# Copies of the first two attention states on ACT instead of DVE, and the four chunk scans of the late stabiliser at other unit ends

## What is computed

```python
for t in range(S):
    m_new = np.maximum(f_gate[:, :, t] + m, i_gate[:, :, t])
    f_stab, i_stab = np.exp(f_gate[:, :, t] + m - m_new), np.exp(i_gate[:, :, t] - m_new)
    C = f_stab * C + i_stab * outer(v_t, k_t);  n = f_stab * n + i_stab * k_t
    y[:, :, t] = o * (C q_t) / np.maximum(abs(n . q_t), 1.0)
x  = (silu(xn @ w_gate) * (xn @ w_val)) @ w_out        # xn: RMS-normalised y, d_ff = 1536
out = (sigmoid(x @ w_gate2) * (x @ w_val2)) @ w_out2
```

## Time and profile before

| | us |
|---|---|
| median of three runs | 469.57 |
| the profiled execution | 469.45 |
| its span | 467.7 |
| PE busy | 458.5 |
| DVE busy | 226.1 |
| ACT busy | 184.6 |
| POOL busy | 26.8 |

### The profile page before, as it was taken

How to read it: one execution, slowest core, us unless ns; L and a number is a source line. 1 busy time by engine, 2 the same in 40 slices (tenths; PEclk the granted TensorE clock), 3 DMA queues, 4 the chain that set the end, 5 groups by cost and what they waited for, 6 DMA issues and landing times.

```text
span 467.7 us, 7890 instructions
## 1 busy us (share of the span) xinstructions
PE 458.5 (98%) x3067; PEld 378.0 (81%) x3067; DVE 226.1 (48%) x451; ACT 184.6 (39%) x379; POOL 26.8 (6%) x59
## 2 busy tenths in 40 slices
PE   8899999999999999999999999999999999999997
PEld 4588898888888887888888888888888888888885
DVE  5898658876666553645555452222322222322222
ACT  6755546553542342354444552222322222322222
POOL 4411111111010000000000000000000000000000
PEclk9999999999999999999999999999999999999999
DMA  7565026620210300002222200000000000100001
GB/s 217 186 193 145 22 96 204 178 86 15 72 36 24 125 2 0 2 1 95 95 97 95 83 0 0 2 0 1 32 24 1 0 1 0 57 1 0 1 0 57
DMA packets 15837, 26.30 MB, mean 56 GB/s; under 512 B 2264, under 2 KB 10808, under 8 KB 15800
## 3 DMA queue, kind: packets, MB, share of 16 engines
q1 hardware_dynamic: 15576, 25.68, 17.7%
q10 hardware_dynamic: 224, 0.12, 0.1%
HBM read 23.55 MB, written 1.97 MB: 55 GB/s over the span
## 4 chain that ended last, share of the span: by engine, by line
PE 90%; DVE 4%; issue 3%; ACT 1%; POOL 1%; DMA 1%; DVEq 0%; POOLq 0%; ACTq 0%
PE bank L1373 53%; PE bank L1435 7%; PE bank L1437 7%; PE bank L1436 7%; PE bank L1443 3%; PE bank L1444 3%; PE pair L1313 2%; PE pair L1290 2%; PE bank L1380 1%; PE pair L1327 1%; PE pair L1279 1%; PE bank L1345 1%; PE bank L1360 1%; DMA fi_row<-fi_first 1%; DVE x_lo L1027 0%
## 5 line engine op out<-in xcount | busy, mean ns | idle before, releaser
L1373 PE MATMUL bank<-x_hi,gv_split 128*128 128x512 f32 (+1 forms) x780 | 236.6, 374 | 1.4 <-DVE hid L1052 0.8
L1373 PEld LDWEIGHTS bank<-x_hi,gv_split 128*128 128x128 f32 x780 | 143.1, 188 | 28.2 <-issue 2.4
L1373 PE MATMUL bank<-x_lo,gv_split 128*128 128x512 f32 (+1 forms) x436 | 161.4, 373 | 0.0
L1065 DVE TENSOR_TENSOR hid<-hid,bank 128x512 f32<-128x512 f32 x48 | 33.0, 687 | 132.4 <-PE bank L1373 132.4
L625 ACT ACTIVATE hid_hi<-hid 128x512 fp32r<-128x512 f32 (+1 forms) x78 | 46.6, 598 | 123.0 <-DVE hid L1065 90.6
L1373 PEld LDWEIGHTS bank<-x_lo,gv_split 128*128 128x128 f32 x436 | 82.0, 188 | 14.1
L618 ACT ACTIVATE hid<-bank 128x512 f32<-128x512 f32 (+1 forms) x78 | 43.9, 562 | 119.1 <-PE bank L1373 88.7
L1072 DVE TENSOR_TENSOR hid_lo<-hid,hid_hi 128x512 fp32r<-128x512 f32 (+1 forms) x78 | 51.1, 655 | 42.1 <-ACT hid_hi L625 42.1
L1435 PE MATMUL bank<-hid_hi,wo_split 128*128 128x512 f32 (+1 forms) x154 | 59.7, 388 | 0.0
L1437 PE MATMUL bank<-hid_hi,wo_split 128*128 128x512 f32 (+1 forms) x154 | 57.5, 374 | 0.0
L1436 PE MATMUL bank<-hid_lo,wo_split 128*128 128x512 f32 (+1 forms) x154 | 57.5, 373 | 0.0
(11 more groups left out here) (165 smaller groups left out, 358.0 us busy)
## 6 DMA issues: line engine op xcount, KB each, us to landing
gv_raw<-wgv SPq DMA_DIRECT2D x24, 384.0 KB, 3.1
qk_tile<-qk SPq DMA_DIRECT2D x24, 160.0 KB
wo_raw<-wo SPq DMA_DIRECT2D x24, 160.0 KB, 3.2
v_sb<-v SPq DMA_DIRECT2D x12, 168.0 KB, 4.6
gate<-og SPq DMA_DIRECT2D x12, 160.0 KB, 3.5
k_sb<-k SPq DMA_DIRECT2D x10, 160.0 KB, 4.7
outT<-y_out SPq DMA_DIRECT2D x6, 256.0 KB, 2.0
rhs<-log_split SPq DMA_DIRECT2D x16, 4.0 KB
```

The costliest lines, as they stand in the source:

```text
L1065: ins = nc.vector.tensor_tensor(h, h, v_ps[:, 0:size], ALU.mult)
L1373: mm = pe.matmul(ps[:, 0:size], lhs, rhs, start=(i == 0), stop=whole and i == len(passes) - 1)
```

## The change

DVE no longer copies states 0 and 1; ACT does it with an activation of kind Copy. `first_state(0)` stands in unit 0 behind round_hidden(0) and before round_wo(1); `first_state(1)` stands in unit 1 behind activate(1) and before gate_tanh(2). The scans of chunks 2, 3, 4, 5 stand at the ends of units 1, 1, 3, 3 instead of 0, 0, 1, 3. All that stands ahead of unit 0 is the same.

```diff
-SCAN_AT = (0, 0, 1, 3)
+SCAN_AT = (1, 1, 3, 3)
...
+            def first_state(t):
+
+                act.wait_ge(st_done, t + 1)
+                nc.scalar.activation(state[t][:], st_ps[:, 0:HG * DV].rearrange("p (h d) -> p h d", h=HG),
+                                     ACT.Copy).then_inc(state_done, 1)
...
                 activate(u)
+                if u == 1:
+                    first_state(1)
...
                     round_hidden(u)
+                if u == 0:
+                    first_state(0)
...
                 sums = st_ps[:, 0:HG * DV].rearrange("p (h d) -> p h d", h=HG)
-                if t < B:
-                    nc.vector.tensor_copy(state[t][:], sums).then_inc(state_done, 1)
-                else:
-                    dve.wait_ge(decayed, t - B + 1)
-                    dve.wait_ge(att_out, 2 * t + 2)
-                    nc.vector.tensor_tensor(state[t % B][:], sums, faded[:], ALU.add).then_inc(state_done, 1)
+                dve.wait_ge(decayed, t - B + 1)
+                dve.wait_ge(att_out, 2 * t + 2)
+                nc.vector.tensor_tensor(state[t % B][:], sums, faded[:], ALU.add).then_inc(state_done, 1)
...
-                if u == 1:
-                    update_state(1)
...
-                if u == 0:
-                    update_state(0)
```

## The result

The changed kernel takes 468.85 us in the median (468.73 to 469.08), the kernel before 469.52 in the runs made beside it; the ratio is 0.9984, 95% interval 0.9978 to 0.9990. That is 0.67 us less. The forecast was 0.5 us less (469.1 us; 0.25 to 0.7 won). The interval leaves out 1, so the changed kernel is the faster one, but by about 0.15% only, less than the 0.2% that the prediction held to be tellable. The profiled span went from 467.7 to 467.0 us.

The account below looks back on a forecast made before the run. DVE sets the pace from 26 to 48 us, then PE alone. Unit 6 starts at 51.22 instead of 51.80, 0.58 us won; less 0.1 for collisions, 0.5: 469.57 - 0.5 = 469.07, written 469.1 us, range 468.4 to 469.8.

Parts of the forecast that it names:

- The frame: Start of unit 6 on PE: how much earlier it comes is the change's worth; everything behind it moves along.
- Part 1: Copies leave DVE: 0.2 us won at state 0, about 0.06 at state 1; PE 0.88 earlier, called the larger gain.
- Part 2: Copies on ACT: 0.35 us each, bounds 0.2 and 0.4, both covered by ACT's waiting and so costing nothing.
- Part 3: Two first scans leave unit 0, a 0.90 us step on DVE: combine(2) at about 30.75, 0.95 us earlier.
- Part 4: Ends of units 1 and 3, one scan more each: 0.50 us hidden in unit 1's following hole, 0.50 given back in unit 3.
- Part 5: Unit 6 on PE: the later of PE's arrival, 51.15, and the x_hi path, 51.22, counts; gain 0.58 us.
- What can eat some of it: POOL's unit 1 instructions and DVE's with two SBUF inputs hold each other up: 0.1 us taken off the gain.
- DVE first: At 28.85 DVE's rest_gv(2) gets in before POOL's fade: it ends at 29.7 and nothing is lost.
- (a): Slower: DVE's gain, under 0.30 us at combine(2), does not arrive, the second scan's cost does; 469.9 us; chance 0.10.
- (b): Nothing measurable: POOL first at both places and longer handovers, about 0 to 0.2 us won; 469.5 us; chance 0.11.
- (c): 0.95 us or more won: unit 3's 0.50 hidden too, the 0.2 ahead of unit 6 gone; 468.5 us; chance 0.09.
- (d): Granted clock falls as PE's hole ahead of unit 5 grows to 1.27 us; 10 us at 1.2 GHz cost 5; chance 0.03.

## Why the prediction was right, and where not

**The frame** held: only the start of unit 6 on PE counts. It was forecast at 51.22 and came at 51.15, and everything behind it moved along: PE's last product starts at 463.44 instead of 464.07. One reading was wrong: units 1 to 4 have two holes of 0.99 us on DVE and not one. The second, ahead of rest_hidden(4), stands behind gate_hidden(4) and so changed nothing in the sum, but it is where the last scan belongs.

**Part 1** was right on what goes away and wrong on what it is worth. "The larger gain is PE's" is the sentence that failed: the copies alone won 0.00 us, since PE's 0.88 us turned into a wait for combine(2) and POOL's earlier fade took the 0.2 us that DVE had won, and the moved scans alone removed the 0.88 too. I had counted the wait where it showed, at the copy, and not asked what stood ahead of the copy in DVE's list: mostly the two scans. The sum of the prediction did not use the 0.88; it went by combine(2), and so the forecast did not suffer. The copy of state 0 was worth 0.16 and not 0.2 (weigh_scores(2) at 26.26 instead of 26.42), that of state 1 0.05, close to the 0.06 (from gate_hidden(1) to value_hidden(1) 0.51 instead of 0.56).

**Part 2** was right. The copies last 0.29 and 0.32 us on ACT, within the bounds of 0.2 and 0.4 and a little under the 0.35 taken; the wait ahead of activate(1) shrank from 0.68 to 0.47, and PE did not notice.

**Part 3** was right to the hundredth: combine(2) at 30.75, waiting for PE, and 0.95 us arrived. That DVE has to wait there shows in the step: 0.48 from value_hidden(1) to combine(2) instead of 0.33.

**Part 4** was right in its sums: gate_hidden(2) at 36.10, rest_hidden(2) at 37.52, gate_hidden(4) at 47.12 against 47.08. The hole did pay for the 0.50. What the prediction did not say is that it could not have paid for more: the 0.5 that were left were no reserve, as the extra scan showed with 0.37 us. So the 0.50 fitted the free 0.51 by luck.

**Part 5** was right in its way: the later of the two conditions is x_lo of block 3, behind PE's turn and x_hi. X_lo ends at 50.18 + 0.87 = 51.05, unit 6 starts 0.10 behind it, and before the change it was the same 0.10 (51.70 and 51.80). The list of waits no longer shows it, because the profile counts a wait from the end of PE's last product (50.78 + 0.28 = 51.06). But from the start of that product to the next one it takes 0.37 us here, and 0.12 where nothing is waited for (36.64 to 36.76), so PE still waits some 0.25 us. The runs with the extra scan at the ends of units 1 and 3 have the same 0.10 (51.35 and 51.45, 51.44 and 51.54). So the condition that the prediction called PE's own arrival, 51.15 by its sum, was too late by these 0.25, and that it equals the measured start is chance.

The term that was mis-sized is the way from the gate products of unit 5 to x_hi. The forecast moves the gate products by 0.45 and x_hi by 0.58. They moved by 0.41 (48.06 to 47.65) and 0.66 (49.92 to 49.26). Of the 0.25 gained between them, 0.13 were in the sum: the handover from the turn to x_hi is 0.10 instead of 0.23. The other 0.12 are PE's turn of block 3. It ended at 49.69 before: it started at 49.14, 0.05 behind the end of ACT's scaling, and its row was 0.55 us long (the same 0.05 and 0.55 stand in the run with the last scan ahead of rest_hidden(4), 48.49, 48.54). So it waited for the scaling, as far as starts and ends tell; now it follows its neighbour with a step of 0.12 instead of 0.18 and takes 0.49, and ends at 49.16. From x_hi to unit 6 it is 1.89 us, 1.88 forecast. So the pure sum was 0.58 and the trace has 0.65.

**What can eat some of it** took off 0.1 us more, which did not come. Of the two collisions that it names, that of the fade was there, but in the changed kernel it cost DVE nothing. DVE's rest_gv(2), which waited first, went ahead of the fade: 1.50 us, ended at 29.84, as in the case "DVE first". What the collision of rest_gv with the weighting costs was in the sum already, since line 1044 had lost as much before (0.97 instead of 0.41). Had the order been the other one, the 0.15 us that combine(2) waits for PE (30.60 by its list) would have taken a part of it; this is worked out and not run. POOL's root beside the second scan, 35.96, did not wait. So 0.63 to 0.67 was won and not 0.5. That the fade can cost 0.2 us is shown by the copies alone, where the scans stood behind rest_gv.

**The rivals**: (a) did not come: it needed combine(2) less than 0.30 us earlier, and it came 0.95 earlier. (b) and (c) neither. (c)'s idea, to hide the 0.50 at the end of unit 3, came true in part by another place for the last scan, and gave 0.91 us. (d) did not come: the granted clock stayed at 1.00 from 40 to 50 us, with a hole of 1.29 us.

## What to carry to other kernels

A wait in the list is charged to the instruction that ended it, but what it costs is all that stands ahead of that instruction in its engine's list; ask what is next for the waiter, or the gain only changes its name. A hole in a busy engine's list has a fixed part, the way through another engine and back, and a free part: work ahead of the first step uses only the free part, while work inside the gap can use all of it. Before a helper engine is released earlier, look at what it will then run beside.

## What the runs showed of the hardware

POOL and DVE hold each other up when POOL reads SBUF and DVE's instruction takes both its inputs from SBUF, and they take turns. The order was first come, first served in these rows. The weighting, issued at 28.07 with DVE's line 1051 running from 28.00 to 28.41, lasted 0.96 us instead of 0.76. Rest_gv(2), issued at 28.34, then lasted 1.50 instead of 0.94 and ended 0.81 after the weighting (29.84 and 29.03). The fade, issued at 28.99, lasted 1.18 instead of 0.47 and ended at 30.17.

The Trainium skill ("SBUF — State Buffer", the section "SBUF: two separate sides") tells of such an exclusive lock for a whole instruction. These rows agree that the other one stands still, and add that the one that waits first goes next. They do not bear out the whole instruction, if that is the length of its row. Rest_gv ended 0.81 after the weighting's row, where it needs 0.94 by itself. And in the run with the scan ahead of rest_hidden(2) the fade, issued at 37.12, lasted 0.58 instead of 0.46, though the scan's row went on to 37.44: it was held 0.12 us and not 0.32.

An instruction of DVE with one input in PSUM was not touched: gate_hidden(1) at 29.76, beside the fade, took 0.41 us, as it did at 29.91 with the scans moved only, where POOL stood still. POOL's root of 128x1 and a scan did not hinder each other: 0.56 and 0.97 us for two, as apart.
